# Expert output product in three passes of rounded two-part operands, and where the dense weights are split

## The reference

```python
for e in range(E):
    mask = expert_idx == e
    h = np.maximum(x[mask] @ w1[e], 0.0)
    out[mask] = gate_w[mask, None] * (h @ w2[e])
...
h = x @ w_in
g = np.maximum(h, 0.0) + alpha * np.minimum(h, 0.0)
return (g @ w_out).astype(np.float32)
```

## Time and profile before

| | us |
|---|---|
| median of 3 runs | 1079.62 (1074.36 to 1083.18) |
| the profiled execution's own time | 1077.54 |
| its span, first to last instruction | 1075.2 |
| attention and routing | 0 to about 396 |
| expert stage, first product to last output copy | 398.0 to 698.1 |
| dense stage | 700.3 to 1075.2 |
| mean granted TensorE clock | 0.987 of full |

### The profile page before, as it was taken

The page is one execution under the profiler, slowest core; times in us unless marked ns, Lnnn a source line. Parts: engine busy times, 40 slices in busy tenths (PEclk is TensorE's granted clock), DMA queues, the critical chain, the costliest instruction groups (busy, mean ns, idle before and its releaser), DMA issues. The chain is left out here.

```text
span 1075.2 us, 47391 instructions
## 1 busy us (share of the span) xinstructions
PE 972.3 (90%) x21177; PEld 849.6 (79%) x21178; DVE 604.9 (56%) x981; ACT 316.3 (29%) x737; POOL 288.3 (27%) x351
## 2 busy tenths in 40 slices
PE   3436779999999999999999999979999999999997
PEld 3425778888888857887878888758999999999997
DVE  8997959898988651111111111156666566656654
ACT  5535636655555501010101101031221222222211
POOL 1019989899800012116511000060101000000000
PEclk9999979999999999999999999999999999999999
DMA  7967858888888359986874644130010101010100
GB/s 235 263 185 207 219 146 241 259 256 256 250 255 239 109 171 305 286 292 220 238 263 165 177 165 166 62 104 1 25 25 25 26 1 25 1 25 2 25 1 25
DMA packets 118303, 159.60 MB, mean 148 GB/s; under 512 B 68468, under 2 KB 87812, under 8 KB 117860
## 3 DMA queue, kind: packets, MB, share of 16 engines
q1 hardware_dynamic: 103956, 125.12, 38.3%
q0 software_dynamic: 5824, 25.28, 8.0%
q10 hardware_dynamic: 8464, 8.43, 2.4%
HBM read 133.15 MB, written 19.23 MB: 142 GB/s over the span
## 5 line engine op out<-in xcount | busy, mean ns | idle before, releaser
L1098 DVE TENSOR_SCALAR ht<-h_bank 128x512 f32<-128x512 f32 x62 | 42.7, 691 | 233.1 <-PE h_bank L1075 226.2
L1361 ACT CAST g_hi<-g 128x512 fp32r<-128x512 f32 x96 | 59.5, 620 | 282.3 <-DVE g L1315 277.9
L1086 PE MATMUL y_bank<-w_all,ht 128*128 x496 | 138.8, 433 | 0.4 <-DVE ht L1098 0.3
L1230 PE MATMUL y_bank<-w_out_hi,g_hi 128*128 128x320 f32 x380 | 118.3, 311 | 3.3 <-DVE g_lo L1295 3.3
L1086 PEld LDWEIGHTS y_bank<-w_all,ht 128*128 128x128 f32 x496 | 91.8, 190 | 35.2 <-issue 0.9
L1075 PE MATMUL h_bank<-xt,w 128*128 128x128 f32 x992 | 119.0, 278 | 0.0
L1230 PE MATMUL y_bank<-w_out_hi,g_lo 128*128 128x320 f32 x380 | 117.8, 310 | 0.0
L1230 PE MATMUL y_bank<-w_out_lo,g_hi 128*128 128x320 f32 x380 | 117.5, 309 | 0.0
L1075 PEld LDWEIGHTS h_bank<-xt,w 128*128 128x128 f32 x992 | 113.1, 192 | 3.8
L1217 PE MATMUL h_bank<-xt_hi,w_in_hi 128*128 128x512 f32 x288 | 114.3, 397 | 0.5 <-DVE xt_hi L1278 0.5
L1217 PE MATMUL h_bank<-xt_hi,w_in_lo 128*128 128x512 f32 x288 | 112.9, 392 | 0.0
(11 more groups left out here) (207 smaller groups left out, 1751.6 us busy)
## 6 DMA issues: line engine op xcount, KB each, us to landing
w<-w_in SPq DMA_DIRECT2D x31, 1024.0 KB
t_in<-wab_in SPq DMA_DIRECT2D x24, 776.0 KB, 4.4
t_in<-wak_in SPq DMA_DIRECT2D x24, 776.0 KB, 6.1
w_all<-w_in POOLq DMA_DIRECT2D x8, 1280.0 KB, 9.9
rr<-rr_in SPq DMA_DIRECT2D x24, 384.0 KB
w_rest<-w_in SPq DMA_DIRECT2D x62, 128.0 KB
vt<-vt_in SPq DMA_DIRECT2D x24, 256.0 KB
vtm<-vtm_in SPq DMA_DIRECT2D x24, 240.0 KB, 3.1
```

What stands on the lines that cost most here:

```text
L1086: last = pe.matmul(y_bank[s][:, 0:FEAT], ht[s][:, f, :], w2[:, ds(e * W2 + f * FEAT, FEAT)], start=f == 0, stop=f == NF - 1)
L1098: dve.tensor_scalar(ht[s][:, FH * n:FH * n + FH, :].rearrange("q f t -> q (f t)"), h_bank[s][n][:, :], 0.0, None, ALU.max).then_inc(s_relu, 1)
L1230: last = pe.matmul(y_bank[n][:, 0:FEAT], g_part[j % RING][:, n * PARTS:(n + 1) * PARTS], v[:, f, :], start=f == 0 and p == 0, stop=f == NF ...
L1361: act.copy(g_hi[j % RING][:, :], g[j % 2][:, :]).then_inc(s_ghi, 1)
```

## The change

**Output product of the experts.** The relu output and w2 of the tile's expert are each held in two rounded parts. ScalarE makes `ht_hi` (relu and rounding in one activation per half), VectorE `ht_lo` (relu minus the high part). ScalarE copies the expert's w2 in four parts of 640 columns into `w2_hi`, VectorE makes `w2_lo`. Both w2 buffers exist once; each part waits until the output product of the tile before has used it (`s_used`). TensorE does 24 products of 320 columns instead of 8 in full precision.

**Order in the expert stage.** TensorE's order becomes: hidden product of tile t+1, transposes of tile t+2, output product of tile t. VectorE's: low part of the hidden values of t+1, repetition of x of tile t+3, low part of w2 for t+1. ScalarE's: high part of the hidden values of t+1, copy of the transposes of t+2, high part of w2 for t+1, output copy of t. ScalarE and VectorE now read the expert's number; TensorE no longer does.

**w_in.** GpSimd loads it straight into `keep.w_in`, with no split and no wait, and the gathers keep their places between the loads. The dense stage splits it in 16 slices of 128 hidden features (3 x 128 columns each): ScalarE `high_w`, VectorE `low_w`, two slices ahead of the w_out parts and the others one per step of the first block. The output buffers `y` of the dense stage now lie in `keep.w_in`. In `attention`, one semaphore of the routing is merged into another.

```diff
@@ -976,20 +977,27 @@
         m = Memory(nc, ctx)
         two = (0, 1)
         NK, NF = len(KT), FF1 // PARTS
+        PIECES = 4
+        FP = NF // PIECES
         w1, w2, x, s_w1, s_w2, s_x = keep.w1, keep.w2, keep.x, keep.s_w1, keep.s_w2, keep.s_x
         xt = [m.sb(f"xt5_{s}", [PARTS, NK, ET]) for s in two]
-        ht = [m.sb(f"ht{s}", [PARTS, NF, ET]) for s in two]
+        ht_hi, ht_lo = ([m.sb(f"{n}{s}", [PARTS, NF, ET], F32R) for s in two] for n in ("ht_hi", "ht_lo"))
+        w2_hi, w2_lo = (m.sb(n, [PARTS, NF, FEAT], F32R) for n in ("w2_hi", "w2_lo"))
         y = [m.sb(f"y5_{s}", [PARTS, FEAT]) for s in two]
         t_bank = m.bank("t_bank")
         h_bank = [[m.bank(f"h_bank{s}{n}") for n in two] for s in two]
         y_bank = [m.bank(f"y_bank{s}") for s in two]
         FH = NF // 2
-        w_raw = m.sb("w_raw", [PARTS, FF2])
-        s_dense, s_raw, s_split = (m.sem(n) for n in ("s_dense", "s_raw", "s_split"))
-        s_t, s_xt, s_h, s_relu, s_y, s_yout = (m.sem(n) for n in ("s_t5", "s_xt5", "s_h5", "s_relu5", "s_y5", "s_yout5"))
+        s_dense = m.sem("s_dense")
+        s_t, s_xt, s_h, s_hthi, s_htlo, s_w2hi, s_w2lo, s_used, s_yout = (m.sem(n) for n in (
+            "s_t5", "s_xt5", "s_h5", "s_hthi5", "s_htlo5", "s_w2hi5", "s_w2lo5", "s_used5", "s_yout5"))
         s_store = [m.sem(f"s_store5{s}") for s in two]
         s_dup = m.sem("s_dup")
...
+        def known(tile, limit):
+
+            return not isinstance(tile, int) or tile < limit
 
...
+        def expert_of(eng, tile):
+            return eng.value_load(keep.owner[0:1, ds(tile, 1)], min_val=0, max_val=EXPERTS - 1)
+
+        def half(t, n):
+            return t[:, FH * n:FH * n + FH, :].rearrange("q f t -> q (f t)")
+
+        def piece(t, p):
+            return t[:, FP * p:FP * p + FP, :].rearrange("q f t -> q (f t)")
+
+        def of_expert(e, p):
+            return w2[:, ds(e * W2 + p * FP * FEAT, FP * FEAT)]
...
             pool.wait_ge(s_w2, 16 * EXPERTS)
-            link = chain(pool, s_split)
             for k, (k0, kn) in enumerate(KT):
                 for first in range(0, PARTS, kn):
-                    pool.dma_start(w_raw[first:first + kn, :], inp["w_in"][k0:k0 + kn, :]).then_inc(s_raw, 16)
-                pool.wait_ge(s_raw, 16 * (k + 1 if kn == PARTS else k + 2))
-                link(pool.tensor_copy(keep.w_hi[:, k, :], w_raw[:, :]))
-                link(pool.tensor_tensor(keep.w_lo[:, k, :], w_raw[:, :], keep.w_hi[:, k, :].bitcast(F32), ALU.subtract))
+                    pool.dma_start(keep.w_in[first:first + kn, k, :], inp["w_in"][k0:k0 + kn, :]).then_inc(s_dense, 16)
                 for tile in range(XRING + 2 + 4 * k, XRING + 6 + 4 * k):
                     gather(tile)
             pool.dma_start(keep.w_out[:, :, :], inp["w_out"].rearrange("(n q) f -> q n f", q=PARTS)).then_inc(s_dense, 16)
             pool.dma_start(keep.slope[:, :], inp["slope"]).then_inc(s_dense, 16)
             for tile in range(XRING + 2 + 4 * len(KT), NET):
                 gather(tile)
-            pool.wait_ge(s_dense, 16 * 2)
+            pool.wait_ge(s_dense, 16 * (len(KT) + 1 + 2))
...
+            pe.sem_inc(s_used, PIECES)
...
 
-            def body(i, c, tile):
+            def hidden(i, c, tile):
                 s = c % 2
-                e = pe.value_load(keep.owner[0:1, ds(tile, 1)], min_val=0, max_val=EXPERTS - 1)
                 pe.wait_ge(s_w1[s], 48 * (XRING // 2 * i + c // 2 + 1))
-
-
                 pe.wait_ge(s_xt, tile + 1)
                 for f in range(FH):
                     for h in two:
@@ -1076,35 +1090,59 @@
                                              xt[s][:, k, :], start=False, stop=f == FH - 1 and k == 1)
                     last.then_inc(s_h, 1)
 
-                if not (isinstance(tile, int) and tile + 1 == NET):
-                    transposes((c + 1) % XRING, tile + 1)
-                pe.wait_ge(s_w2, 16 * (e + 1))
+            def outputs(c, tile):
+                s = c % 2
                 pe.wait_ge(s_yout, tile + 1)
-                for f in range(NF):
-                    if f % FH == 0:
-                        pe.wait_ge(s_relu, 2 * tile + f // FH + 1)
-                    last = pe.matmul(y_bank[s][:, 0:FEAT], ht[s][:, f, :], w2[:, ds(e * W2 + f * FEAT, FEAT)],
-                                     start=f == 0, stop=f == NF - 1)
-                last.then_inc(s_y, 1)
+                pe.wait_ge(s_htlo, 2 * tile + 2)
+                for p in range(PIECES):
+                    pe.wait_ge(s_w2lo, PIECES * tile + p + 1)
+                    for f in range(FP * p, FP * p + FP):
+                        for n, (h, w) in enumerate(((ht_hi, w2_hi), (ht_hi, w2_lo), (ht_lo, w2_hi))):
+                            last = pe.matmul(y_bank[s][:, 0:FEAT], h[s][:, f, :], w[:, f, :],
+                                             start=f == 0 and n == 0, stop=f == NF - 1 and n == 2)
+                    last.then_inc(s_used, 1)
+
+            def body(i, c, tile):
+                if known(tile, NET - 1):
+                    hidden(i, c + 1, tile + 1)
+                if known(tile, NET - 2):
+                    transposes((c + 2) % XRING, tile + 2)
+                outputs(c, tile)
             transposes(0, 0)
+            hidden(0, 0, 0)
+            transposes(1, 1)
             rings(pe, body)
 
         @block.vector
         def _(dve):
-            def body(i, c, tile):
+            def low_h(c, tile):
                 s = c % 2
                 for n in two:
-                    dve.wait_ge(s_h, 2 * tile + n + 5)
-                    dve.tensor_scalar(ht[s][:, FH * n:FH * n + FH, :].rearrange("q f t -> q (f t)"), h_bank[s][n][:, :],
-                                      0.0, None, ALU.max).then_inc(s_relu, 1)
-                if not (isinstance(tile, int) and tile + 2 >= NET):
-                    repeated(i + (c + 2) // XRING, (c + 2) % XRING)
+                    dve.wait_ge(s_hthi, 2 * tile + n + 1)
+                    dve.scalar_tensor_tensor(out=half(ht_lo[s], n), in0=h_bank[s][n][:, :], scalar=0.0, in1=half(ht_hi[s], n).bitcast(F32),
+                                             op0=ALU.max, op1=ALU.subtract).then_inc(s_htlo, 1)
+
+            def low_w2(tile):
+                e = expert_of(dve, tile)
+                for p in range(PIECES):
+                    dve.wait_ge(s_w2hi, PIECES * tile + p + 1)
+                    dve.tensor_tensor(piece(w2_lo, p), of_expert(e, p), piece(w2_hi, p).bitcast(F32), ALU.subtract).then_inc(s_w2lo, 1)
 
             def repeated(i, c):
                 dve.wait_ge(s_x[c], 16 * (i + 1))
                 dve.tensor_copy(x[c][:, FEAT:], x[c][:, 2 * PARTS:FEAT]).then_inc(s_dup, 1)
-            for c in two:
+
+            def body(i, c, tile):
+                if known(tile, NET - 1):
+                    low_h(c + 1, tile + 1)
+                if known(tile, NET - 3):
+                    repeated(i + (c + 3) // XRING, (c + 3) % XRING)
+                if known(tile, NET - 1):
+                    low_w2(tile + 1)
+            for c in range(3):
                 repeated(0, c)
+            low_h(0, 0)
+            low_w2(0)
             rings(dve, body)
...
+            def high_h(s, tile):
+                if known(tile, 0) or tile >= 2:
+                    act.wait_ge(s_used, PIECES * tile)
+                for n in two:
+                    act.wait_ge(s_h, 2 * tile + n + 5)
+                    act.activation(half(ht_hi[s], n), h_bank[s][n][:, :], ACT.Relu).then_inc(s_hthi, 1)
+
+            def high_w2(tile):
+                e = expert_of(act, tile)
+                act.wait_ge(s_w2, 16 * (e + 1))
+                for p in range(PIECES):
+                    act.wait_ge(s_used, PIECES * tile + p + 1)
+                    act.copy(piece(w2_hi, p), of_expert(e, p)).then_inc(s_w2hi, 1)
+
             def body(i, s, tile):
-                static = isinstance(tile, int)
-                if not (static and tile + 1 >= NET):
-                    turned(1 - s, tile + 1)
-                act.wait_ge(s_y, tile + 1)
+                if known(tile, NET - 1):
+                    high_h(1 - s, tile + 1)
+                if known(tile, NET - 2):
+                    turned(s, tile + 2)
+                if known(tile, NET - 1):
+                    high_w2(tile + 1)
+                act.wait_ge(s_used, PIECES * tile + 2 * PIECES)
                 act.wait_ge(s_store[s], 16 * (i + 1))
                 act.copy(y[s][:, :], y_bank[s][:, 0:FEAT]).then_inc(s_yout, 1)
                 act.wait_ge(s_yout, tile + 3)
                 act.dma_start(dram["expert_out"][ds(tile * ET, ET), :], y[s][:, :]).then_inc(s_store[s], 16)
             turned(0, 0)
+            high_h(0, 0)
+            turned(1, 1)
+            high_w2(0)
             tiles(act, body)
...
-        y = [m.sb(f"y6_{s}", [PARTS, SUB, FEAT]) for s in two]
+        w_hi, w_lo = (m.sb(n, [PARTS, NK, FF2], F32R) for n in ("w_in_hi", "w_in_lo"))
+        SPLIT, V_LATE = 2, {2: 0, 3: 3}
```

(33 more changed lines are left out.)

23 lines of the change are left out of this document (13 added, 10 removed).

## The result

The changed kernel takes 1060.68 us (median of 4 runs, 1054.93 to 1068.94) against 1076.99 us for the kernel before on the same chip (1073.99 to 1083.18): ratio 0.9869, 95% interval 0.9825 to 0.9913, so 1.3% faster. The forecast was 1061.0.

A forecast was written before the change was run, and what follows sets the result against it. TensorE was taken to set the pace, DMA second. Expert stage -19.6 and dense stage +1.0 gave -18.6 us: the profiled 1077.5 becomes 1058.9, and with 2.1 for the median 1061.0; range 1050 to 1073.

The forecast's parts named there:

- Part 1: Expert output product: 24 rounded products take 3.52 us instead of 4.40, saving 27.3 us over 31 tiles.
- Part 2: Expert-stage splits: 5.0 us a tile on ScalarE, 4.9 on VectorE, hidden under 8.62; no cost, no table reloads.
- rival D: Expert stage: no gain from the products, or ScalarE/VectorE is the bound; 1081 us, chance 0.09.
- Part 3: Expert-stage order and loads: late gather 10 delays outputs(8) by 7.0 us; stage ends at 678.0, 19.6 us less.
- the lower clock: Expert stage: TensorE runs slower after its pause for tile 10's x, 1.8 us (0 to 3.6).
- w1: Expert stage: w1 loads landing late, 2 us (0 to 6).
- rival B: Expert stage: w1 late, the DMA limit holding ten tiles of w_in and w_out loads at 9.50 us; 1068, chance 0.13.
- the x wait: Expert stage: VectorE waits 10 to 16 us for x of tile 10, TensorE idle 7 us near 480 to 487.
- Part 4: Dense stage: splitting 16 slices of w_in there adds 1.0 us (0 to 4).
- Rival A: Expert stage: the x wait hardly exists; 25 us less, 1054.5, chance 0.20.
- C: Expert stage: w2 loads starved by w1, gather 10 landing 27 us after the forecast's time; slower, 1088, chance 0.06.

The follow-up runs named there:

- order_only: The changed kernel with the output product as before (full precision, no splits of relu and w2); 1084.67 us, ratio 1.0060 to the kernel before.
- no_w2_split: The changed kernel, but from tile 1 on the copies and subtractions of w2 take 8 columns instead of 640; 1069.07 us.
- again: The changed kernel unedited, a second set of runs with a second profile; 1056.08 us, ratio 0.9817 to the kernel before.
- after: The first profiled run of the changed kernel, the slowest of its set; 1068.94 us.
- paced: The changed kernel with GpSimd's w_in and w_out loads spread out between later gathers; 1049.94 us, ratio 0.9754 to the kernel before.
- early_x: The changed kernel with tiles 8, 9 and 10 gathered earlier among the w2 loads, w_in still in a burst; 1058.57 us, ratio 0.9841.
- Start_x: The changed kernel with spread w_in and w_out loads, earlier gathers of tiles 8 to 10, and tile 1 gathered before the first w2 load; 1044.61 us.
- dense_only: The kernel before with only the change's dense stage and w_in loaded straight to its place; 1081.20 us, ratio 1.0018 to the kernel before.
- before_again: The kernel before, unedited, run once and profiled a second time; 1086.37 us.

## Why the prediction came out

The time, 1060.7 against 1061.0, is closer than the working deserves, since errors of both signs met. By its own steps:

**Part 1** held in kind, not quite in size: a tile gains 0.79 us and not 0.88, 24.5 us in all instead of 27.3. The row it rested on (12 in 1.76) stands between products of 128 rows, and so could not show the 0.09 us of the step to the 64-row products, which the 4.40 us of the old product did contain. Order_only shows that the products alone carry the gain.

**Part 2** held: durations within 0.02 us, one table load, and no_w2_split shows the cover. The rival D (products bring nothing, or the engines bound) is out.

**Part 3** held for the chain (10.49 us a load instead of 10.65, outputs(8) 89.8 and 90.1 us after the first hidden product instead of 88.4). From there to the last output copy the run again needs 191.7 us (281.5 - 89.8) where 191.6 was forecast (678.0 - 486.4), partly by luck: the lower clock took 1.4 us of its 1.8 (outputs(8) lasts from 486.77 to 491.83, 5.06 us for 3.70) and w1 0.4 of its 2, and the 0.09 us that each of 23 tiles takes beyond the forecast, 2.1 in all, filled the place. (The 12.45 us that the prediction gives w1 add up to 12.47; nothing hangs on it.) Two terms were mis-sized, and one was missing:
- w1, "2 (0 to 6)": in after 2.75 + 5.06 us of waits and some 4.6 us of lower clock behind them (0.77 + 0.82 at 477.21, 0.92 + 2.10 at 511.93), together 12.4; in again 1.6. This is rival B's mechanism, in one execution of two, but not its cause. B reckoned with the mean demand of ten tiles; paced shows that the demand is met, and that the three thirds of w_in in 12 us are what makes the long wait. That the thirds would close up once their splits were gone was in the diff, but the prediction asked only when the gather behind the first third would land. They don't always make it: of six profiles with the burst three have a w1 wait of 4 to 5 us behind it (after, early_x, order_only), and in again the x wait covered it. The 2.75 us with 1.6 of clock come before the burst, and their cause stays open. The Trainium skill (DMA: Bandwidth & Descriptors, Queues, rings and completion order) has each DMA engine go round robin between queues, from which the prediction had 8.7 us for a w1 load beside w2; the load issued at 493.96 landed only shortly before 511.93, some 18 us, so an even share between two queues doesn't describe the burst. What the shares are no run shows.
- the x wait of VectorE was 11.55 us in again (forecast 10 to 16), but TensorE lost 3.32 + 0.81 = 4.1 us for it and not 7: tiles had already come later by 2.0 us from the start, 1.3 from w1 and the quiet tile's 0.09 us each. In after it lost 1.4, since w1 had held it up before. Delays in a row hide each other, and their sum is steadier than its terms.
- missing: the start. The prediction let hidden(1) begin at 405.3, when outputs(0) did before, and run at full clock; its x came in behind the first w2 load. From the first hidden product to the third tile's it counted 7.3 + 8.6 = 15.9 us, after and again took 17.9, of which 1.6 (10.30 for 8.71) are the lower clock. Start_x wins it back.

**Part 4** was +1.0, and measured -3.1 (363.9 to 360.8). The term itself was about right. Its main piece shows singly: outputs(1), which waited 0.30 us for g_lo, waits 0.77 to 0.84 in all ten profiles with the new dense stage, about 0.5 more where 0.56 was reckoned. And the three kernels with the new dense stage that stall in step 2 as the kernel before does (dense_only 364.9, order_only 365.2, no_w2_split 363.6, mean 364.6) are 1.4 above before and before_again (363.9, 362.4, mean 363.2), within the spread of either. But in after and again that stall is absent, 3.8 us with its clock (364.6 - 360.8). The last section has it.

In sum, against -18.6 of the forecast: expert stage -19.6 forecast, -18.1 in again and -11.4 in after; dense stage +1.0 forecast, -3.1 in both; all of it against one profile of before, and against before_again the expert stage gained 23.4 and 16.7. The misses of opposite sign are what brought the sum so near. Rival A is out by its mechanism and not by its 25 us, which the second set's interval all but reaches: the x wait was there, 11.55 us. C, starved w2, is out too, since the w2 loads took 10.5 us on average, where C needed 13.3.

## What to carry to other kernels

Where a change takes a slow step out of a queue, write down when every transfer behind that step now starts, not only the one that is known to be late: the step may have been what spaced them, and spacing them by hand (one large load every two tiles) was worth 4 to 6 us here by the medians of two pairs of kernels. When one wait is taken away and the time stands still, look for the next gate at the same place before giving up the remedy: early_x alone gave nothing, and the spacing together with a gather moved at the start gave the best kernel. Price a new order and a new operation by kernels that have only one of them; their sum alone (-20 us) hides one of about -26 us, and beside it perhaps one of +4.
